# Reordering the first stretch of a fused attention and expert kernel, with TensorE working on ones ahead of it

## What is computed

```python
attn = softmax(q @ mean8(k).T / 8) @ mean8(v)       # 8 batches, 8 heads, 576 rows, 72 pooled keys
x = attn rows as (4608, 512)
h = ((x @ w1) * (x @ w2)) @ w3                      # 512 -> 1024 -> 1024
x = h @ w_out                                       # 1024 -> 512
logits = x @ w_gate + modality_bias[modality_id]    # 8 experts, the best one is taken
out = gate * (relu(x @ e_w1[expert]) @ e_w2[expert])
```

## Time and profile before

| what | us |
|---|---|
| median of 3 runs | 1208.62 (1207.16 to 1209.24) |
| the profiled execution itself | 1206.19 |
| its span, first to last instruction | 1204.3 |
| TensorE busy | 1184.0 (98% of the span) |
| VectorE, ScalarE, GpSimd busy | 522.1, 265.8, 212.3 |
| mean granted TensorE clock | 0.996 of full |

### The profile page before, as it was taken

How to read it: one execution, slowest core, us unless ns; L and a number is a source line. 1 busy time by engine, 2 the same in 40 slices (tenths; PEclk the granted TensorE clock), 3 DMA queues, 4 the chain that set the end, 5 groups by cost and what they waited for, 6 DMA issues and landing times.

```text
span 1204.3 us, 26009 instructions
## 1 busy us (share of the span) xinstructions
PE 1184.0 (98%) x10806; PEld 1044.8 (87%) x10807; DVE 522.1 (43%) x1159; ACT 265.8 (22%) x518; POOL 212.3 (18%) x245
## 2 busy tenths in 40 slices
PE   7999999999999999999999999999999999999996
PEld 5878888978889788898898989899999899899895
DVE  0746647465474664756413144722222243222221
ACT  1322222222222222222222223211111131111110
POOL 2560222022220221202000001021121112121121
PEclk9999999999999999999999999999999999999998
DMA  9641223132230322303000005052111101111111
GB/s 362 209 163 29 94 86 110 36 92 89 84 112 29 95 93 84 113 28 95 10 28 1 36 1 202 20 178 77 44 61 35 44 26 54 43 45 52 35 51 37
DMA packets 41247, 92.76 MB, mean 77 GB/s; under 512 B 9411, under 2 KB 16707, under 8 KB 40132
## 3 DMA queue, kind: packets, MB, share of 16 engines
q1 hardware_dynamic: 32308, 66.68, 16.5%
q0 software_dynamic: 6400, 20.50, 5.3%
q10 hardware_dynamic: 2448, 4.26, 1.0%
HBM read 70.93 MB, written 21.01 MB: 76 GB/s over the span
## 4 chain that ended last, share of the span: by engine, by line
PE 97%; DMA 1%; DVE 1%; issue 0%; SPq 0%; ACT 0%; POOLq 0%; DVEq 0%
PE ab L700 17%; PE ab L701 17%; PE ab L702 17%; PE rt L700 6%; PE x2p L700 6%; PE x2p L702 6%; PE x2p L701 6%; PE rt L701 6%; PE rt L702 6%; PE sct L764 3%; PE ab L713 2%; PE ab L786 2%; PE sct L859 1%; PE rt L713 1%; PE x2p L713 1%; DMA wo_x<-in_moe_w_out 1%
## 5 line engine op out<-in xcount | busy, mean ns | idle before, releaser
L701 PE MATMUL ab<-xtl,e1h 128*128 128x256 f32 x608 | 170.5, 280 | 0.0
L700 PE MATMUL ab<-xth,e1h 128*128 128x256 f32 x608 | 169.5, 279 | 1.0 <-issue 1.0
L702 PE MATMUL ab<-xth,e1l 128*128 128x256 f32 x608 | 169.3, 278 | 0.0
L1557 DVE SCALAR_TENSOR_TENSOR htl<-ab,hth 128x512 fp32r<-128x512 f32 x76 | 52.3, 691 | 157.1 <-ACT hth L1127 157.0
L1127 ACT ACTIVATE hth<-ab 128x512 fp32r<-128x512 f32 x76 | 45.3, 597 | 339.4 <-PE ab L702 339.4
L700 PE MATMUL ab<-xh,w1h 128*128 128x512 f32 x288 | 116.0, 403 | 1.5 <-DVE xl L1208 1.5
L1225 DVE TENSOR_TENSOR ac<-ab,ac 128x512 f32<-128x512 f32 x72 | 49.8, 691 | 152.8 <-PE ab L702 90.8
L700 PEld LDWEIGHTS ab<-xth,e1h 128*128 128x128 f32 x608 | 114.1, 188 | 2.0 <-issue 1.4
L701 PEld LDWEIGHTS ab<-xtl,e1h 128*128 128x128 f32 x608 | 114.4, 188 | 0.7
L702 PEld LDWEIGHTS ab<-xth,e1l 128*128 128x128 f32 x608 | 114.2, 188 | 0.0
L701 PE MATMUL ab<-xl,w1h 128*128 128x512 f32 x288 | 112.9, 392 | 0.0
(11 more groups left out here) (198 smaller groups left out, 2395.3 us busy)
## 6 DMA issues: line engine op xcount, KB each, us to landing
kv<-in_v SPq DMA_DIRECT2D x24, 512.0 KB, 4.8
qt<-in_q SPq DMA_DIRECT2D x8, 1280.0 KB, 6.2
kv<-in_k SPq DMA_DIRECT2D x16, 576.0 KB, 7.7
x_rows<-xr SPq DMA_DIRECT2D x36, 256.0 KB, 3.1
stage<-in_moe_w SPq DMA_DIRECT2D x8, 1024.0 KB, 9.8
vp<-v_rows SPq DMA_DIRECT2D x32, 192.0 KB, 3.4
w3b<-in_moe_w ACTq DMA_DIRECT2D x16, 256.0 KB, 6.7
wo_x<-in_moe_w_out SPq DMA_DIRECT2D x8, 256.0 KB, 7.0
```

What stands on the lines that cost most here:

```text
L700: pe.matmul(outp, lh, rh, start=first, stop=False)
L701: pe.matmul(outp, lh, rl, start=False, stop=False)
L702: return pe.matmul(outp, ll, rh, start=False, stop=last)
L1557: dve.scalar_tensor_tensor(out=htl[:, fs, :].rearrange("p f n -> p (f n)"), in0=ab[n // 2][:, n % 2, :], scalar=0.0, in1=hth[:, fs, :].rea ...
```

## The change

- TensorE first runs 40 matmuls of a 128x128 table of ones with itself into a bank that nobody reads (`warm_up`).
- The left halves (0,0), (1,0), (2,0) come first, then `wog_turned`, (3,0), `wog`, then the right halves (0,1) to (3,1) with their gate columns; from c = 4 on left and right alternate as before. `lg0` and its copies are gone; all parts have 260 columns. Banks go by the order of the parts.
- w_out comes in 8 transfers: four of the left 260 columns (two blocks of 128 rows each, runs of 1040 bytes) before w_out transposed, four of the right 252 (runs of 1008 bytes) after it.
- ScalarE's queue issues w3 block 0, w_gate, waits until the first half of block 0 has landed, then issues blocks 1 to 3.
- The rounds of scores stand before (3,1), (4,0), (4,1), (5,1) and (6,0); (7,1) is cut in two, and the second half of `weigh_v` stands in its middle. ScalarE's and VectorE's orders follow; `hi_w12` goes through the blocks in the order 0, 1, 4, 2, 5, 6, 3, 7.
- GpSimd subtracts w2's first block (4) before it pools the third part of v; SP waits for that and issues block 6 ahead of the store of v's third part, and block 7 after the spread.
- In the first expert step VectorE runs `decode()` ahead of `lo_xt(1, ...)`.

```diff
-W12_WITH = {2: (1, 2), 3: (3, 4), 4: (5,), 5: (6,), 6: (7,)}
+LEFT = 4
+WARM = 40
+W12_ORDER = (0, 1, 4, 2, 5, 6, 3, 7)
+ROUND_BEFORE = {(3, 1): 0, (4, 0): 1, (4, 1): 2, (5, 1): 3, (6, 0): 4}
...
-        def load_wo(engine, f):
-            engine.dma_start(wo_x[:, f, 0:DM], moe_w_out[:, f, :]).then_inc(wo_in[f], 16)
+        def load_wo(engine, part, n):
+            fs, cols = slice(2 * n, 2 * n + 2), slice(XH * part, min(DM, XH * (part + 1)))
+            engine.dma_start(wo_x[:, fs, cols], moe_w_out[:, fs, cols]).then_inc(wo_in[part][n], 16)
...
+        def w34_no(c, part):
+            return LEFT * part + c + 1 if c < LEFT else 2 * c + part + 1
+        def start_bank(no):
+            return (ab1[:, 0, :], ab1[:, 1, :], x2p, rt)[(no - 1) % 4][:, 0:XH]
...  SP
                 store_v(b, 1)
+                if before_last:
+                    before_last()
                 store_v(b, 2)
                 spread_v(b)
...
-            for f in range(FC):
-                load_wo(sp, f)
+            for n in range(FC // 2):
+                load_wo(sp, 0, n)
             load_wo_t(sp, 0)
             load_wo_t(sp, 1)
+            for n in range(FC // 2):
+                load_wo(sp, 1, n)
...
-            bring_v(0, late_w12)
-            for c in range(W12_DVE + 2, 2 * KC):
+            def next_w12(c):
                 sp.wait_ge(w12l_late, c - W12_DVE - 1)
                 load_w12(sp, c)
+            bring_v(0, late_w12, lambda: next_w12(W12_DVE + 2))
+            next_w12(W12_DVE + 3)
...  GpSimd
-            pool_kv(0)
+            for m in range(2):
+                pool_k(0, m)
+            for m in range(2):
+                pool_v(0, m)
+            lo_w12_late(W12_DVE)
+            pool_v(0, 2)
+            for c in range(W12_DVE + 1, 2 * KC):
+                lo_w12_late(c)
...  TensorE
+            def warm_up():
+                pe.wait_ge(pool_done, 1)
+                for n in range(WARM):
+                    pe.matmul(sct[:, 0, 0:P], ones[:, :], ones[:, :], start=True, stop=True)
...
+            def w34_part(c, part, fs=range(FC)):
+                no = w34_no(c, part)
+                if no > 4 and fs[0] == 0:
+                    pe.wait_ge(w34h_ready, no - 4)
+                    pe.wait_ge(w34l_ready, no - 4)
+                for f in fs:
                     if part == 0 and f % 4 == 0:
                         pe.wait_ge(w3_in[c % W3_BUFS][f // 4], 16 * (c // W3_BUFS + 1))
+                    if c == 0 and f % 2 == 0:
+                        pe.wait_ge(wo_in[part][f // 2], 16)
...
             def first_w34():
-                w34_part(0, 0)
-                w34_part(0, 1)
+                warm_up()
+                for c in range(LEFT - 1):
+                    w34_part(c, 0)
                 wog_turned()
-                w34_part(1, 0)
+                w34_part(LEFT - 1, 0)
                 wog()
                 pe.wait_ge(wog_ready, 1)
-                lg0()
-                w34_part(1, 1)
+                for c in range(LEFT):
+                    score_before(c, 1)
+                    w34_part(c, 1)
...
-            for c in range(2, FC):
-                if c < FC - 1:
-                    may_score(0, c - 2)
-                    score(c - 2)
-                w34_part(c, 0)
-                if c == FC - 1:
-                    weigh_v(0, 0)
-                w34_part(c, 1)
+            for c in range(LEFT, FC - 1):
+                for part in range(2):
+                    score_before(c, part)
+                    w34_part(c, part)
+            w34_part(FC - 1, 0)
+            weigh_v(0, 0)
+            w34_part(FC - 1, 1, range(0, FC // 2))
             weigh_v(0, 1)
+            w34_part(FC - 1, 1, range(FC // 2, FC))
...  ScalarE
-            load_w3(act, 0, 0)
+            for half in range(2):
+                load_w3(act, 0, half)
             act.dma_start(wg[:, :, :], w_gate).then_inc(wg_in, 16)
-            load_w3(act, 0, 1)
-            for half in range(2):
-                load_w3(act, 1, half)
+            act.wait_ge(w3_in[0][0], 16)
+            for c in range(1, W3_BUFS):
+                for half in range(2):
+                    load_w3(act, c, half)
...  VectorE, first expert step
             lo_ht(0, [3])
+            decode()
             lo_xt(1, 1, 1, None)
-            decode()
             step_tables()
```

More of the change, by code:

```diff
@@ L302, in build @@
         xl_ready = sem("xl_ready")
-        wo_in = [sem(f"wo_in{n}") for n in range(FC)]
+        wo_in = [[sem(f"wo_in{part}_{n}") for n in range(FC // 2)] for part in range(2)]
         w3_in = [[sem(f"w3_in{n}_{half}") for half in range(2)] for n in range(W3_BUFS)]
@@ L402, in load_w12, with w34_cols @@
             engine.dma_start(w12_raw(c), (w1_v if c < KC else w2_v)[c % KC]).then_inc(w12_in[w12_slot(c)], 16)
[L404 to L409, removed]
+        def w34_no(c, part):
+            return LEFT * part + c + 1 if c < LEFT else 2 * c + part + 1
+        def start_bank(no):
+            return (ab1[:, 0, :], ab1[:, 1, :], x2p, rt)[(no - 1) % 4][:, 0:XH]
+        def w34_cols(part):
+            return slice(XH * part, XH * (part + 1))
         def x2_bank(n):
@@ L733, in wog, with score_before @@
                 mm.then_inc(wog_done, 1)
[L735 to L738, removed]
             def first_w34():
-                w34_part(0, 0)
-                w34_part(0, 1)
+                warm_up()
+                for c in range(LEFT - 1):
+                    w34_part(c, 0)
                 wog_turned()
-                w34_part(1, 0)
+                w34_part(LEFT - 1, 0)
                 wog()
                 pe.wait_ge(wog_ready, 1)
-                lg0()
-                w34_part(1, 1)
+                for c in range(LEFT):
+                    score_before(c, 1)
+                    w34_part(c, 1)
+            def score_before(c, part):
+                if (c, part) in ROUND_BEFORE:
+                    may_score(0, ROUND_BEFORE[c, part])
+                    score(ROUND_BEFORE[c, part])
             def may_score(b, m):
@@ L1054, in exp_gate @@
                 act.activation(gx[:, :, :], dl[:, :, :], ACT.Exp).then_inc(gx_ready, 1)
[L1057 to L1060, removed]
+            for c in range(LEFT - 1):
+                hi_w34(c, 0)
             act.wait_ge(wog_t_done, 1)
             act.activation(wog_t[:, 0, :], ab0[:, 0, :], ACT.Copy).then_inc(wog_t_taken[0], 1)
-            hi_w34(1, 0)
+            hi_w34(3, 0)
             hi_wog()
-            hi_lg0()
+            hi_w34(0, 1)
             bring_w3(4)
+            hi_w34(1, 1)
+            bring_w3(5)
             hi_w12(0)
[L1068 to L1076, removed]
+            hi_w34(2, 1)
+            bring_w3(6)
+            exp_p(0, 0)
+            hi_w12(1)
+            hi_w34(3, 1)
+            bring_w3(7)
+            exp_p(0, 1)
+            hi_w12(4)
+            hi_w34(4, 0)
+            exp_p(0, 2)
+            hi_w12(2)
+            hi_w34(4, 1)
+            hi_w12(5)
+            hi_w34(5, 0)
+            hi_w12(6)
+            exp_p(0, 3)
+            hi_w34(5, 1)
+            hi_w12(3)
+            exp_p(0, 4)
+            hi_w34(6, 0)
+            hi_w12(7)
+            hi_w34(6, 1)
+            hi_w34(7, 0)
             hi_x(0, 0)
-            hi_w34(FC - 1, 1)
             hi_x(0, 1)
+            hi_w34(7, 1)
             def hi_xt(t):
@@ L1333, in _ @@
             dve.wait_ge(dve_done, own.next())
-            lo_w34(0, 0)
-            lo_w34(0, 1)
+            for c in range(LEFT - 1):
+                lo_w34(c, 0)
             dve.wait_ge(wog_t_done, 2)
             dve.tensor_copy(wog_t[:, 1, :], ab0[:, 1, :]).then_inc(wog_t_taken[1], 1)
-            lo_w34(1, 0)
-            lo_lg0()
+            lo_w34(3, 0)
             dve.wait_ge(pad_stored, 32)
[L1341 to L1350, removed]
+            lo_w34(0, 1)
+            lo_w34(1, 1)
+            lo_w34(2, 1)
+            lo_w12(0)
+            soft_max(0, 0)
+            soft_sum(0, 0)
+            lo_w34(3, 1)
+            soft_turn(0, 0)
+            soft_max(0, 1)
+            soft_sum(0, 1)
+            soft_turn(0, 1)
+            lo_w34(4, 0)
+            soft_max(0, 2)
+            soft_sum(0, 2)
+            lo_w34(4, 1)
+            soft_turn(0, 2)
+            lo_w12(1)
+            lo_w12(2)
+            lo_w34(5, 0)
+            soft_max(0, 3)
+            soft_sum(0, 3)
+            lo_w34(5, 1)
+            soft_turn(0, 3)
+            soft_max(0, 4)
+            soft_sum(0, 4)
+            lo_w34(6, 0)
+            soft_turn(0, 4)
+            lo_w34(6, 1)
+            lo_w12(3)
+            lo_w34(7, 0)
             lo_x(0, 0)
-            lo_w34(FC - 1, 1)
             lo_x(0, 1)
+            lo_w34(7, 1)
             dve.wait_ge(w12l_late, 2 * KC - W12_DVE)
```

55 lines of the change are left out of this document (17 added, 38 removed).

## The result

The changed kernel took 1214.49 us (median of 8 runs, 1211.89 to 1217.92), the kernel before on the same chip 1208.89 (8 runs, 1207.16 to 1213.08): ratio 1.0045, 95% interval 1.0026 to 1.0063. It is slower by 0.45%. The forecast was 6.5 us faster, and its range of 1199.4 to 1205.3 missed. The profiled execution took 1212.9 us (span 1210.8, clock 0.994), 6.7 more than the 1206.19 of before.

The account below looks back on a forecast made before the run. TensorE's work plus idle time was taken as the bound. Head: 69.2 + 6.0 + 0.5 + 0.8 + 0.3 = 76.8, against 83.80; 7.0 less 0.5 for decode gives 6.5 us, 1202.1 against the median; range 1199.4 to 1205.3.

Parts of the forecast that it names:

- Moved, at nothing: Head: VectorE's and ScalarE's new orders, SP's wait for GpSimd and the third part's later pooling cost no time.
- nothing in the end: Rival: mid-head bound by VectorE or ScalarE, score rounds waiting 0.8 us or more for softmax; 1206.5 or over; chance 0.04.
- Start of the real work: Head start: shorter w_out runs delay TensorE's real work by 0.7 us, to 6.0; bounds 5.4 and 6.6.
- rule of whole packets: Rival, head start: engines drain whole packets of one queue before switching, start stays at 5.4; 1201.3; chance 0.07.
- Warm-up: Head start: the ones bring the clock up before real work; 0.5 us lost, bounds 0 and 3.
- Late blocks: Left halves: 0.8 us of waits for w3 blocks 1 to 3, bounds 0 and 2.5; as rival 1204.1, chance 0.14.
- Clock behind `wog`: Head: light stretch shrinks from 3.97 to 2.1 us, clock stays full; other bound 1.76 us lost.
- (7,1) cut in two: Head's end: wait before first dense product covered, new one of 0.3 us ahead of second `weigh_v`; bounds 0 to 1.
- decode: First expert step: `decode` ahead of `lo_xt` makes the step tables later, 0.5 us lost; bounds 0 and 0.5.
- The round trip of v: Rival, head: v pooled and spread later than `weigh_v` wants it at 69.5; v at 78.5 gives 1211; chance 0.02.
- The range: Whole kernel: 1199.4 with all new losses at 0, to 1205.3 with late blocks or the clock with another us.

Follow-up runs that it names:

- even rounds: The changed kernel with score rounds two parts apart, at most one w1 block between two rounds on VectorE, ScalarE's order to match, `decode` back: 1203.88 us, ratio 0.9980.
- the cold run: The changed kernel without the 40 matmuls of ones, profiled in a single run: 1210.24 us.
- the change again: The changed kernel itself, timed again as yardstick for the run without ones: 1213.55 us, ratio 1.0052 to the kernel before.
- its timed cold run: The changed kernel without the 40 matmuls of ones, timed beside the change itself: 1213.19 us, ratio 1.0052 to the kernel before.
- decode back: The changed kernel with `decode()` behind `lo_xt(1)` again in the first expert step: 1214.66 us.
- block 1 early and cold: Even rounds, with ScalarE's queue issuing w3 block 1 without waiting for block 0's first half, and without the ones: 1203.40 us, ratio 0.9968.
- the last: Block 1 early and cold, with GpSimd pooling k of batch 2 only after VectorE's seventh `gl` of batch 0: 1200.12 us, ratio 0.9944.
- the run where GpSimd waits: The changed kernel, but GpSimd begins its last three w2 blocks only when VectorE has done three of w1: 1207.3 us (one run).
- the order run: The changed kernel with VectorE's low parts of w1 blocks 1 and 2 moved behind the fifth softmax: 1207.69 us, ratio 1.0009.

## Why the prediction was wrong

**The step that failed** is "Moved, at nothing": "banks are waited for four parts (14 us) later, scores need a softmax of 1.5 us done one part before". It looked at what each operation needs, and not at the queue that it stands in. In the kernel before VectorE was idle ahead of four of the five softmaxes (1.06 to 5.80 us); the new order has four rounds within 18 us (36.74 to 54.52) and two blocks of w1 behind them, and from 37.3 to 74.6 us VectorE's only idle times of note are five of 0.75 us behind ScalarE's exponentials. And it gave GpSimd's work beside VectorE's no price. "Nothing in the waits now speaks for it" was true and no reason: a wait that an order creates cannot stand in the trace of another order. The rival "nothing in the end" named the place, at a chance of 0.04.

**What it cost**, in the profiled change. The head ended at 86.22, 9.4 us after the 76.8 forecast: 6.18 and 0.64 are waits of rounds for VectorE, 9.01 - 7.28 + 1.26 - 0.89 = 2.1 the half clock behind the first of them, 0.5 all the rest. Behind the head 4.0 us were lost, where 0.5 were forecast: 1.1 at `x2p`, 0.55 by `decode`, 1.26 without a cause in the records, the rest in steps of 0.35 and less. Without the order that failed (even rounds) the head ended at 77.75, 0.95 after the forecast.

**Start of the real work**: forecast 6.0, it came at 5.24 to 5.79 in all runs of this w_out layout, in most nearer the lower bound of 5.4. By the Trainium skill ("DMA: Bandwidth & Descriptors", Queues, rings and completion order), whose rule of whole packets gave 5.4, this would be so; the runs agree with the number and don't show the mechanism. In the change the ones themselves ended only then (1.10 + 4.32 = 5.42) and no wait for data stands there; the four runs without ones, which did wait for w_out, began at 5.24, 5.37, 5.57 and 5.77. The working had slipped too: 2.1 against 1.3 us is 0.8, which makes 6.2.

**Warm-up**: clock full when real work starts (0 of 0.5 lost), (0,0) in 4.4 us with its wait. But the gain did not reach the sum: against the cold run (0,0) ended 0.8 us earlier, and (1,0), which waits for block 1 of w3, started at the same time. The bound of 3 us lost without a warm clock was not there to be saved in this kernel.

**Late blocks**: forecast 0.8, measured 1.4 (0.26 + 1.14) in the first profile, and 1.3 to 3.2 for block 1 alone in the others of this queue order with ones; behind the two longest, 2.24 and 3.16, the clock fell. The cause was right; the size was up to four times the 0.8, and what hangs on it was not in the term.

**Clock behind `wog`**: forecast to stay full. It did in seven of the eleven profiles with the changed parts, and fell in four (the change again, its timed cold run, decode back, block 1 early and cold). What decides is open; 1.7 us hang on it, run by run.

**(7,1) cut in two**: a wait of 0.21 us in the change and 0.49 with even rounds, 0.3 forecast. **decode**: 0.5 forecast, 0.53 measured. **The round trip of v** cost nothing: no `weigh_v` waited for `vp` in any run. **The range**: its upper end, the late blocks with another us, adds up to 1205.1, not 1205.3.

**A coupling that was not in the sum at all**: `x2p` near 130 us. GpSimd starts on k of batch 2 when the transfer lands, and that fell onto the last `gl` or just behind it. In the kernel before, k was pooled 8.1 us after its issue (122.25 to 130.39) and the wait was 0.66; in the change 7.0 us after (124.82 to 131.83), and 1.74. Over all other runs but the last it was 0.35 to 2.5: any shift of the head rolls this again.

## What to carry to other kernels

When an order of work is changed, add up each helper engine's queue between two of TensorE's needs, and with the durations that it has beside its busiest neighbour, not its median ones: two subtractions of 1.2 us that took 2.9 each made a 6 us wait here, of which their place in the queue alone was 2.7. Such a wait costs more than its length where the clock falls behind it (2.1 us behind 6.18), so an earlier start that only runs into late data is not free: ahead of data-bound work, warm-up made this kernel no faster and once slower. Profile a kernel whose runs spread more than once, and compare the granted clock beside each time before putting a difference down to the edit.

## What the runs showed of the hardware

**VectorE and GpSimd hold each other up as whole instructions.** In the change a VectorE multiply of 0.75 us started at 48.42 beside a GpSimd subtraction that ran from 48.18 for 2.35 us:

```profile
48.42 2.72 DVE L1221 TENSOR_TENSOR pb<-pb,rc 128x576 f32<-128x576 f32 x1
```
```profile
48.18 2.35 POOL L616 TENSOR_TENSOR w2l<-w_late,w2h 128x1024 fp32r<-128x1024 f32 x1 [7.47 <-ACT w2h L1027]
```

It ended at 51.14: 50.53, GpSimd's end, plus its own time, less 0.1. The subtraction of `mx` from the scores, whose input lies in PSUM, kept its 0.76 us throughout, in all runs. This is what the Trainium skill states ("SBUF — State Buffer", Who interferes with whom): a VectorE instruction with two SBUF inputs contends with a GpSimd instruction that reads SBUF, and the second to start is blocked until the first ends. The runs agree with it, the order of the two included. In the kernel before, a w1 and a w2 subtraction met as well, but VectorE was first by 0.09 us: it took its usual 1.18, and GpSimd took 3.31 in place of 2.35 (timeline of before):

```profile
53.48 1.18 DVE L1169 TENSOR_TENSOR w1l<-w_early,w1h 128x1024 fp32r<-128x1024 f32 x1
53.57 3.31 POOL L610 TENSOR_TENSOR w2l<-w_late,w2h 128x1024 fp32r<-128x1024 f32 x1 [3.08 <-ACT w2h L1009]
```

In the same kernel with ones GpSimd began 1.3 us ahead of the same block, and VectorE took 2.57. So a row of 1.18 us from the trace of before was no price for another order. I had not weighed it, although it spoke against this change: by these rows a GpSimd subtraction of w2 that began before VectorE's costs VectorE 1.4 to 2.2 us, and the change set two blocks of w1 behind the start of two of them. The tiny operation of 1.44 us in the run where GpSimd waits has one input, which that sentence doesn't cover.

**The fall of the clock is a matter of the run.** The same program, the kernel before with ones, ran at a granted clock of 0.997 in one execution and at 0.993 or 0.994 in five, 3 to 5 us longer. Falls stood behind repeated waits of 0.5 to 0.7 us, behind single waits of 2.08 us and more, and behind the small matmuls of `wog`, but not each time behind each: the short execution had six waits of 0.39 to 0.69 us at the start, and `x2p`'s wait was 2.44 us in the order run, and no fall followed.
